# A feed-forward split into two phases, with h through DRAM and one level of Strassen's algorithm in its first product

## The reference, cut to what matters

```python
kv = einsum('bhsd,bhse->bhde', k, v); out = einsum('bhsd,bhde->bhse', q, kv)
x = out / sqrt(mean(out * out, -1) + 1e-6) * g_norm        # to (8, 576, 512)
u = x + ((x^T @ U) @ V)^T                                  # rank 32, over the tokens
x2 = u + relu(u @ w_ch1) @ w_ch2                           # 512 -> 2048 -> 512
h = gelu(x2 @ w_in); a, v = halves(h)                      # 512 -> 2 x 512
v_s = w_sg @ (layernorm(v) * g_ln) + b_sg                  # over the tokens
y = x2 + (a * v_s) @ w_out
```

## Time and profile before

| | |
|---|---|
| median of three runs | 1407.95 us |
| the profiled execution | 1410.83 us, span 1409.0 us |
| PE busy | 1376.5 us, 98% |
| DVE busy | 499.2 us, 35% |
| ACT busy | 377.9 us, 27% |
| mean granted TensorE clock | 0.991 of full |
| moved by DMA | 108.40 MB, mean 77 GB/s |

### The profile page before, as it was taken

The page is one execution under the profiler, slowest core; times in us unless marked ns, Lnnn a source line. Parts: engine busy times, 40 slices in busy tenths (PEclk is TensorE's granted clock), DMA queues, the critical chain, the costliest instruction groups (busy, mean ns, idle before and its releaser), DMA issues.

```text
span 1409.0 us, 18444 instructions
## 1 busy us (share of the span) xinstructions
PE 1376.5 (98%) x7342; PEld 1190.5 (84%) x7342; DVE 499.2 (35%) x888; ACT 377.9 (27%) x717; POOL 80.2 (6%) x73
## 2 busy tenths in 40 slices
PE   4799999999999999999999999999999999999998
PEld 4688888888888888888888888888998998998987
DVE  3545233233233232232242211216625426326322
ACT  4534222232232232232232111114323223233221
POOL 2200000000000000000000001001110111102100
PEclk8899999999999999999999999999999999999999
DMA  6454233233223223233222030103220220220211
GB/s 168 133 147 149 53 103 104 57 98 104 62 95 107 62 95 112 52 97 111 51 89 94 25 103 0 61 0 111 74 75 30 57 75 22 63 74 15 71 38 38
DMA packets 144244, 108.40 MB, mean 77 GB/s; under 512 B 93552, under 2 KB 110064, under 8 KB 144176
## 3 DMA queue, kind: packets, MB, share of 16 engines
q1 hardware_dynamic: 141488, 105.31, 24.5%
q10 hardware_dynamic: 2688, 2.10, 0.5%
HBM read 69.63 MB, written 35.65 MB: 75 GB/s over the span
## 4 chain that ended last, share of the span: by engine, by line
PE 95%; DVE 2%; SPq 1%; ACT 1%; DMA 0%; POOL 0%; issue 0%; ACTq 0%; DVEq 0%; POOLq 0%
PE ps L976 28%; PE ps L978 28%; PE ps L977 28%; PE ps L981 4%; PE ps L995 2%; PE ps L1003 2%; PE ps L1011 1%; PE ps L1020 1%; PE ps L1211 1%; PE ps L1212 1%; DMA q_raw<-in_q 0%; PE ps L1005 0%; SPq L307 0%; DVE y_hl L759 0%; DVE bn L893 0%
## 5 line engine op out<-in xcount | busy, mean ns | idle before, releaser
L792 DVE SCALAR_TENSOR_TENSOR h_hl<-ps,h_hl 128x512 fp32r<-128x512 f32 x144 | 99.5, 691 | 452.3 <-ACT h_hl L588 452.3
L976 PE MATMUL ps<-u_sb,w_hi 128*128 128x512 f32 x576 | 228.9, 397 | 1.6 <-DVE u_tail L781 1.6
L976 PE MATMUL ps<-h_hl,w_hi 128*128 128x512 f32 x576 | 230.1, 399 | 0.0
L588 ACT ACTIVATE h_hl<-ps 128x512 fp32r<-128x512 f32 x144 | 86.0, 597 | 524.6 <-PE ps L978 524.5
L977 PE MATMUL ps<-u_sb,w_hi 128*128 128x512 f32 x576 | 225.9, 392 | 0.0
L978 PE MATMUL ps<-u_sb,w_lo 128*128 128x512 f32 x576 | 225.7, 392 | 0.0
L978 PE MATMUL ps<-h_hl,w_lo 128*128 128x512 f32 x576 | 225.1, 391 | 0.0
L977 PE MATMUL ps<-h_hl,w_hi 128*128 128x512 f32 x576 | 224.7, 390 | 0.0
L978 PEld LDWEIGHTS ps<-u_sb,w_lo 128*128 128x128 f32 x576 | 109.0, 189 | 23.6
L976 PEld LDWEIGHTS ps<-u_sb,w_hi 128*128 128x128 f32 x576 | 109.3, 190 | 22.9 <-DVE u_tail L781 1.8
L978 PEld LDWEIGHTS ps<-h_hl,w_lo 128*128 128x128 f32 x576 | 108.1, 188 | 24.0
(11 more groups left out here) (136 smaller groups left out, 1999.3 us busy)
## 6 DMA issues: line engine op xcount, KB each, us to landing
uT_scratch<-u_st SPq DMA_DIRECT2D x28, 576.0 KB, 3.2
u_sb<-uT_scratch SPq DMA_DIRECT2D x16, 768.0 KB, 5.2
x2T_scratch<-x_st SPq DMA_DIRECT2D x9, 1024.0 KB, 4.8
x_raw<-x2T_scratch SPq DMA_DIRECT2D x8, 1152.0 KB, 6.3
q_raw<-in_q SPq DMA_DIRECT2D x64, 128.0 KB, 2.8
out<-o_st SPq DMA_DIRECT2D x32, 256.0 KB, 2.3
k_raw<-in_k SPq DMA_DIRECT2D x60, 128.0 KB, 2.7
v_raw<-in_v SPq DMA_DIRECT2D x30, 256.0 KB, 2.9
```

The lines of the kernel that those rows point to most:

```text
L588: nc.scalar.activation(h_hl[:, f % NH, 0, :], ps[:, f % 2], ACT.Relu).then_inc(s_hhi, 1)
L792: nc.vector.scalar_tensor_tensor(h_hl[:, f % NH, 1, :], ps[:, f % 2], 0.0, h_hl[:, f % NH, 0, :].bitcast(F32), ALU.max, ALU.subtract).then ...
L976: mm(dst, ws[0], xs[0], start=first, stop=False)
```

## The change

The feed-forward becomes two phases. In the first (`up_tile`, eight times, one per batch of 576 tokens) h = u @ w_ch1 is formed and written to DRAM before relu; in the second (`down_tile`, nine tiles of 512 tokens) h is loaded again, split by ScalarE and VectorE from SBUF, and multiplied by w_ch2 as before. The first product is done by one level of Strassen's algorithm in Winograd's form: u (512 x 576) and w_ch1 (512 x 2048) are cut into 2 x 2 quarters, and seven products of quarters and of sums of quarters take the place of eight. The seven stationary operands of w_ch1 are made once, the seven moving ones of u per batch (`x_sum`, `x_high`, `x_low`). For each of four groups of hidden chunks there are seven double steps (`idx` 0 to 6); a step is 6 matmuls of 288 columns. A batch has so 4 x 14 = 56 steps, k = 0 to 55. The seven results pass through three pairs of PSUM banks (`BANK`); ScalarE copies the first two to SBUF (`copied`), VectorE combines the others by seven additions (`added`). An addition must be done before its bank pair is written again: that is what `up_step` waits for. The attention of the next batch stands between the steps, one piece after step 0, 2, 4 and so on in a period of 11 steps. In the last batch's phase the two parts of w_ch2 are made. The transposed u is made in one piece of 576 columns, its last matmul having 320 columns and no longer 384.

```diff
-EARLY = 5
+NPAIR = FC // 2
+NI = 7
+NG = NPAIR // 2
+STEPS = 2 * NI * NG
+BANK = (0, 1, 2, 0, 2, 0, 1)
+NADD = 7
...
+QK0, KV0, ATT0, PERIOD = 0, 2, 4, 11
+QK, KV, LOW, UT = 2, 4, 8, 10
+LAST_UT = ATT0 + (HP - 1) * PERIOD + UT
+HALF_UT = ATT0 + PERIOD + UT
...
+def step(k):
+
+    g, rest = divmod(k, 2 * NI)
+    return g, rest // 2, rest % 2
...
-    uT_dram = nc.dram_tensor("uT_scratch", [P, 2, DC, NT], F32, kind="Internal").ap()
+    uT_dram = nc.dram_tensor("uT_scratch", [P, DC, NT], F32, kind="Internal").ap()
+    hT_dram = nc.dram_tensor("hT_scratch", [P, FC, NT], F32, kind="Internal").ap()
...
+        def w1_sums(eng, ops, g):
+            raw = w1_raw[min(g, 1)][:, max(0, 2 * g - 2):max(2, 2 * g), 1]
+            ops.tensor_tensor(raw[:, :, 1], raw[:, :, 4], raw[:, :, 6], ALU.add).then_inc(s_wsum, 1)
+            ops.tensor_tensor(raw[:, :, 4], raw[:, :, 0], raw[:, :, 4], ALU.subtract).then_inc(s_wsum, 1)
+            ops.tensor_tensor(raw[:, :, 2], raw[:, :, 1], raw[:, :, 0], ALU.subtract).then_inc(s_wsum, 1)
+            ops.tensor_tensor(raw[:, :, 5], raw[:, :, 3], raw[:, :, 2], ALU.subtract).then_inc(s_wsum, 1)
...
+            def store_h(t, g):
+                sp.wait_ge(s_ad, NADD * (NG * t + g + 1))
+                for s_ in range(2):
+                    sp.dma_start(hT_dram[:, 2 * g + s_:FC:NPAIR, t * S:(t + 1) * S],
+                                 h_st[:, g % 2, s_].rearrange("p (f a) m -> p f (a m)", f=2)).then_inc(s_hst[g % 2], 16)
...
+            def load_h(j):
+                t, f = divmod(4 * j, FC)
+                if j >= 2:
+                    sp.wait_ge(s_down, DC * 4 * (j - 1))
+                sp.dma_start(h_raw[:, 4 * (j % 2):4 * (j % 2) + 4, :],
+                             hT_dram[:, f:f + 4, t * TT:(t + 1) * TT]).then_inc(s_hl[j % 2], 16)
...
+            def up_tile(t):
+                m = HP * (t + 1)
+                if t:
+                    store_h(t - 1, NG - 1)
+                load_next(m + 1)
+                load_next(m + 2)
+                store_h(t, 0)
+                store_u(t + 1, 0)
...
+            def copied(t, k):
+                g, idx, s_ = step(k)
+                act.wait_ge(s_p, STEPS * t + k + 1)
+                nc.scalar.activation(h_st[:, g % 2, :, 3 * idx, :], ps[:, 2 * BANK[idx]:2 * BANK[idx] + 2, 0:SH], ACT.Copy).then_inc(s_cp, 1)
...
-            def h_low(n, f):
-                dve.wait_ge(s_hhi, n + 1)
...
+            def added(t, k):
+                g, idx, s_ = step(k)
+                c11, c12, c21, c22 = (h_st[:, g % 2, :, i, :] for i in range(4))
+                p = ps[:, 2 * BANK[idx]:2 * BANK[idx] + 2, 0:SH]
+                dve.wait_ge(s_p, STEPS * t + k + 1)
+                if idx == 2:
+                    nc.vector.tensor_tensor(c12, p, c11, ALU.add).then_inc(s_ad, 1)
+                elif idx == 3:
+                    nc.vector.tensor_tensor(c11, p, c11, ALU.add).then_inc(s_ad, 1)
+                elif idx == 4:
+                    nc.vector.tensor_tensor(c21, p, c12, ALU.add).then_inc(s_ad, 1)
+                    nc.vector.tensor_tensor(c12, c12, c22, ALU.add).then_inc(s_ad, 1)
+                    nc.vector.tensor_tensor(c22, c21, c22, ALU.add).then_inc(s_ad, 1)
+                elif idx == 5:
+                    nc.vector.tensor_tensor(c12, p, c12, ALU.add).then_inc(s_ad, 1)
+                else:
+                    nc.vector.tensor_tensor(c21, p, c21, ALU.add).then_inc(s_ad, 1)
...
+            def up_tile(t, par, first=False, final=False):
+                for k in range(STEPS):
+                    g, idx, s_ = step(k)
+                    if idx > 1 and s_ == 1:
+                        added(t, k)
+                    if first and g + 1 < NG and idx in (3, 6) and s_ == 0:
+                        w1_low(2 * g + (2, 3)[idx == 6])
...
+                    r, at_ = hook(k)
+                    if at_ == 1:
+                        sums(m, sq)
+                    elif at_ == QK and r >= 0:
+                        normalise(m)
+                    elif at_ == KV + 1 and r + 1 < HP:
+                        kv_copy(m + 1, BX)
+                    elif at_ == KV + 2:
+                        y_low(m)
+                    elif at_ == LOW + 1:
+                        a_split(m, BX)
...
+                    if k == LAST_UT + 2:
+                        x_sum(t + 1, 1 - par, 2)
+                        x_low(t + 1, 1 - par, 1)
+                    if k == LAST_UT + 4:
+                        x_sum(t + 1, 1 - par, 6)
+                        x_low(t + 1, 1 - par, 2)
+                    if k == LAST_UT + 5:
+                        x_sum(t + 1, 1 - par, 4)
...
+            def up_step(k, t, par, first):
+                g, idx, s_ = step(k)
+                n = NG * t + g
+                if s_ == 0:
+                    if g == 0:
+                        pe.wait_ge(s_xlo, NI * t + idx + 1)
+                    if idx < 3 and not start:
+                        pe.wait_ge(s_ad, NADD * (n - 1) + (6, 7, 3)[idx])
+                    elif idx == 3:
+                        pe.wait_ge(s_cp, 2 * n + 1)
+                    elif idx == 4:
+                        pe.wait_ge(s_ad, NADD * n + 1)
+                    elif idx == 5:
+                        pe.wait_ge(s_ad, NADD * n + 2)
+                    elif idx == 6:
+                        pe.wait_ge(s_cp, 2 * n + 2)
+                dst = ps[:, 2 * BANK[idx] + s_, 0:SH]
+                for c in range(2):
+                    cs = slice(c * P, (c + 1) * P)
+                    ins = product(dst, [w1[g][:, s_, 0, idx, cs], w1[g][:, s_, 1, idx, cs]],
+                                  [x_hi[:, x_slot(idx, par), c, :], x_lo[par][:, idx, c, :]], c == 0, c == 1)
...
+            pe.wait_ge(s_ad, NADD * NG * B)
+            down_tile(0, 0, first=True, later=False)
```

More of the change, by code:

```diff
@@ L80, in at @@
             cursor[0] = end
+        assert end <= 229344, (name, end)
         return t
@@ L399, in load_x2 @@
+            load_w2(0)
+            load_w2(1)
+            store_h(B - 1, 0)
+            up_steps(B - 1, 4 * NI)
+            load_w2(2)
+            load_w2(3)
+            store_h(B - 1, 1)
+            up_steps(B - 1, 6 * NI)
+            load_w2(4)
+            store_h(B - 1, 2)
+            up_steps(B, 0)
+            store_h(B - 1, NG - 1)
+            for n in range(2):
+                sp.wait_ge(s_hst[n], 32 * 2 * B)
+            load_u(1)
             def load_x2(p, par):
@@ L656, in wc_high @@
+            for f in (14, 15):
+                w2_high(f)
             def wc_high(n):
@@ L658, in wc_high, with wc_at, down_tile @@
                 nc.scalar.activation(wc_piece(n, 0), wc_raw[:, n % NWC, :], ACT.Copy).then_inc(s_wchi, 1)
+            def wc_at(t, f):
+                pos = FC * (t - (NTILE - 2)) + f
+                jj, i = divmod(pos - 6, 4)
+                return 3 * jj + i if pos >= 6 and i < 3 and jj < DC else None
+            def down_tile(t, skip=0, last=False):
+                for f in range(skip, FC):
+                    h_high(t, f)
+                    if last and wc_at(t, f) is not None:
+                        wc_high(wc_at(t, f))
+            down_tile(0, skip=NH)
+            with act.Fori(1, NTILE - 2) as t:
+                down_tile(t)
+            down_tile(NTILE - 2, last=True)
+            x2_high(0, 0, first=True)
+            down_tile(NTILE - 1, last=True)
             def evacuate(p, par):
@@ new lines, in last_up_tile @@
+            def last_up_tile(t):
+                for k in range(STEPS):
+                    g, idx, s_ = step(k)
+                    if idx > 1 and s_ == 1:
+                        added(t, k)
+                    if 24 <= k < 38 and k % 2 == 0:
+                        w2_low((k - 24) // 2)
+                    if 42 <= k < 49:
+                        w2_low(7 + k - 42)
+                    if k in (50, 51, 52, 53):
+                        h_low(0, k - 50)
+            last_up_tile(B - 1)
@@ new lines, in wc_at, with down_tile @@
+            def wc_at(t, f):
+                pos = FC * (t - (NTILE - 2)) + f
+                jj, i = divmod(pos - 6, 4)
+                return 3 * jj + i if pos >= 6 and i < 3 and jj < DC else None
+            def down_tile(t, par, loads=0, skip=0, last=False):
+                for f in range(skip, FC):
+                    h_low(t, f)
+                    if last and wc_at(t, f) is not None:
+                        wc_low(wc_at(t, f))
+                    if f == 3 and not skip:
+                        residual(t - 1, 1 - par, loads)
@@ new lines, in up_tile, with down_tile @@
+            def up_tile(t, par, first=False, final=False):
+                for k in range(STEPS):
+                    up_step(k, t, par, first)
+                    if not final:
+                        attention_step(k, t)
+            up_tile(0, 0, first=True)
+            with pe.Fori(0, B // 2 - 1) as i:
+                up_tile(2 * i + 1, 1)
+                up_tile(2 * i + 2, 0)
```

(14 more changed lines are left out.)

839 lines of the change are left out of this document (416 added, 423 removed).

## The result

The changed kernel takes 1503.64 us, median of four runs (1503.11 to 1505.7), against 1408.64 us of the kernel before on the same chip (1407.45 to 1409.93). The ratio is 1.0677, 95% interval 1.0658 to 1.0695: slower by 6.8%. I had forecast 1425, slower by 1.2%. The direction was right and the size far off.

A forecast was written before the change was run, and what follows sets the result against it. TensorE bounds the kernel, busy 98%. Span 1409.0 - 35.5 - 0.8 + 45.5 + 5 + 2.7 - 1 + 1 = 1425.9; on the median 1407.95 + 16.9 = 1425 us, 1.2% slower; range 1396 to 1441, the forecast's own 1412 to 1438.

The forecast's parts named there:

- The gain: First product: 2688 matmuls of 288 columns replace 1728 of 512, 35.5 us less on TensorE.
- The second phase: Second product with operands now loaded from DRAM: no added cost taken, 0 to 1 us per tile, 9 in all, as upper end.
- The start: Prologue up to the first product: both lists followed give 55, a change of -1 us, of -4 to +8.
- J: Theory for the seam-edits run: low-rank factors ahead of the first kv copy delay the start; first product 2 to 3.5 us earlier.
- The first batch: First batch of the first phase: 6.5 us of waits plus 5 (0 to 12) for VectorE's six low parts of w_ch1.
- The loop: Each batch of the first phase: 62.1 us of TensorE work and 6.5 of waits, the k-v piece returning after 68.6.
- Step 12: Low-rank factor's piece: TensorE waits 1.1 us for VectorE's low part of y, behind step 9's additions and kv's copies.
- Batch's end: TensorE waits 2.2 us for the addition of step 53, which stands behind u's sums and low parts on VectorE.
- rival 2: The clock falls to 1.2 GHz after the batch-end wait, costing 1.7 us per batch: 1437 us; chance 0.15.
- The last batch and boundary: Low part of w_ch2 ahead of one addition (0.45), second phase waiting for the last addition (2.25): 2.7 us.
- Rival 1: Cover suffices at the attention pieces, only the batch-end wait stays; 30 us fall away: 1395 us, faster; chance 0.22.
- Rival 3: SyncE's queue: q, k and v loads late behind h's store at a batch's start, up to 10 us: 1435; chance 0.10.

The follow-up runs named there:

- the last kernel: Changed kernel with the list reorderings, earlier loads, GpSimd's sums held back, seam edits and u's last two parts made later: 1401.55 us, 0.9953 of the kernel before.
- the attention-first kernel: Changed kernel with VectorE's attention operations ahead of h's additions, y's low part behind kv's copies, and the two SBUF additions a step later: 1491.12 us.

## Why the prediction was wrong in size

- **The gain, -35.5: right.** Matmuls of 288 columns start 0.1325 us apart in the first phase. The period of the last kernel, 64.0, bounds it from the other side: the forecast for a batch without waits was 62.1. The 1.9 between them are, in its trace, mostly hand-overs of 0.2 us at five pieces and 1.4 at every second batch, where the loop jumps back.
- **The second phase, forecast 0 (0 to 9), measured 32.9: the step that failed most.** I weighed only whether h arrives in time in a steady tile, and there it does: between 690 and 860 us PE has no gap. I did not walk ScalarE's and SyncE's lists through tiles 7 and 8, where the preparation of the third stage had been put ahead of h. That TensorE would wait needed no duration to see: the load of x2 is issued behind a load that waits for the end of tile 7, and tile 8 begins behind x2. The waits in that part run in a circle through three lists. Their length needed one more thing that I had left out: 5.0 of the longest, 20.77, are VectorE's wait for GpSimd.
- **The start, forecast 54.9, measured 61.9.** I saw that the low-rank factors move ahead and called it a gain. They moved ahead of the copy of kv, and cost 4.5 us (J); GpSimd's sums cost another 5.8 of this start, which I had left out altogether. The two add to more than 7.0, so some part of my 55 was too high, and I can't say which. My reading of the start before was off too: 963.47 less 3456 x 0.2267 and 28 x 4.4 is 56.8 and not 55.9, so the term should have been -1.8 and not -1.
- **The first batch, forecast 6.5 + 5 of waits, measured 27.2 above the 62.1.** TensorE is idle for 17.8 of it, and its 71.5 us of busy time are 9.4 above the 62.1, at a mean clock of 0.90. The largest wait is one that I had not walked: 5.81 us for ScalarE's copy of q, behind the high parts of u, and with GpSimd's sums left out it is 0.37. GpSimd is 7 us of this batch in all. The waits on w_ch1's low parts are 1.01 and 3.06 in the trace, so that term, 5, was sound as far as it went. A batch of the loop has 6 us of idle time and 65.7 of busy time; what the first has above that in busy time, 5.8, goes with the low clock at its start, which I gave only to the batch's end.
- **The loop, forecast 68.6, measured 71.6: waits right, base and clock wrong.** Step 12: 1.24 (1.1). Step 14: 0.92 (1.0). Step 25: 0.65 (0.7). Step 36: 0.93 (1.0). Batch's end: 2.10 (2.2). These five come to 5.8 where I had 6.0, each at its place and on the operation named, and moving the operations made the four at attention pieces go. What is missing is rival 2, which I had held apart and gave 0.15: the clock fell at the batch's end, every time. Here it is not an alternative to that wait but its consequence, and belonged into the sum. Its price by the rows: nine matmuls or so at 0.11 more, q's transposes 0.46 more, the matmul behind them 0.17 more, 1.6 us where the rival had 1.7. Hand-overs of 0.2 us at five pieces make 1.0 of the rest, and pieces that take up to 0.1 longer than in the earlier trace rows what is left.
- **The last batch and boundary, forecast 2.7, measured 5.2.** The boundary wait is 2.29 (2.25). Of the rest, 1.6 is the low clock behind the wait at 581.68 (15 matmuls at 0.24), and 0.9 are three breaks of 0.2 to 0.4, of which I had 0.45.
- **Rivals.** Rival 1, cover suffices: refuted at each place. Rival 3, SyncE's queue: not seen in the changed kernel's loop but for single waits, and seen at once, with 1.63 us, when TensorE came earlier. So it was true and hidden.

My range, 1396 to 1441, was worked out around the terms I had walked. None of its ends held a place that I had not looked at. (Its lower end just leaves out rival 1's own 1395, and the attention's share of VectorE's batch adds up to 17 us by its rows and not to 16; neither matters to the result.)

## What to carry to other kernels

When a change reorders a program, walk every engine's list and the DMA queue's through each seam (start, first and last turn of a loop, boundary of phases), not only the steady turn: 58 of the 76 us of this error lay at seams or in GpSimd's work beside them, and that the worst would come was readable without any duration. Work given to an idle GpSimd has a price where VectorE reads two inputs from SBUF. A wait of 2 us on the bounding engine may have to be priced with the low clock behind it, and removing it is priced with what is late next: here v, ScalarE's copy of q and u's low parts stood right behind. And a good idea can be lost in its order: 1503.6 and 1401.6 us are the same operations.

## What was unexpected of the hardware

- VectorE's operations with both inputs in SBUF took 1.8 us for 0.75 and 3.05 for 2.02 while GpSimd was adding from SBUF, and GpSimd's took 1.8 to 3.0 for 1.27. One of 0.68 took 5.67, behind an operation of GpSimd of 5.58. VectorE's with an input in PSUM kept their 0.28. A cast of 128x128 from SBUF took 0.97 for 0.23, and 0.63 beside GpSimd's memsets.
- The clock did not fall behind every wait of 2 us. Behind the batch's end in the changed kernel (2.10 us) it was at the 1.2 GHz level for some 3 us; behind the wait of 2.06 at step 42 in the attention-first kernel the matmuls went on 0.13 apart. What sets the two apart was not tried.
- A wait of 20.77 us was followed by 5.3 us at the lower level, a start of 0.43 us between matmuls of 512 columns where 0.2267 is the rule.
- At every second batch, where the loop jumps back, TensorE shows 1.25 to 1.35 us of idle time that no engine ends, once the waits that covered it are gone.
